# Probabilities turned by VectorE and moved by small transfers, from the thirteenth double on

## What is computed

```python
scores = q @ k.T / 8                  # per batch and head, 576 x 576
# heads 0..3: keys 0..31 back; heads 4..7: every 4th key, 0..124 back
attn = softmax(where(mask, scores, -1e9))
x = attn @ v                          # -> [4, 576, 512]
k = relu(mix(x, mu_k) @ w_k);  v = k * k @ w_v      # mix: with the token before
x = sigmoid(mix(x, mu_r) @ w_r) * v
u = x + (relu(x.T @ w_tok1) @ w_tok2).T             # over the 576 tokens
out = u + relu(u @ w_ch1) @ w_ch2
```

## Time and profile before

| | |
|---|---|
| median of 3 runs | 707.39 us (707.34 to 707.51) |
| profiled execution, its time | 707.65 us |
| profiled execution, its span | 705.9 us |
| TensorE busy | 698.6 us, 99% of the span |
| VectorE busy | 377.5 us, 53% |
| ScalarE busy | 243.2 us, 34% |
| GpSimd busy | 212.8 us, 30% |
| granted TensorE clock | 0.999 of full speed |

### The profile page before, as it was taken

The page is one execution under the profiler, slowest core; times in us unless marked ns, Lnnn a source line. Parts: engine busy times, 40 slices in busy tenths (PEclk is TensorE's granted clock), DMA queues, the critical chain, the costliest instruction groups (busy, mean ns, idle before and its releaser), DMA issues.

```text
span 705.9 us, 13682 instructions
## 1 busy us (share of the span) xinstructions
PE 698.6 (99%) x5469; PEld 624.7 (88%) x5469; DVE 377.5 (53%) x609; ACT 243.2 (34%) x580; POOL 212.8 (30%) x228
## 2 busy tenths in 40 slices
PE   8999999999999999999999999999999999999997
PEld 8878999999999999999988888888788888888886
DVE  6689868687776777776872225321461225411121
ACT  3674563635445463636441122111231122211110
POOL 5584655756464664735045000000000000000000
PEclk9999999999999999999999999999999999999999
DMA  9941333222322220131912221303112121300011
GB/s 176 297 113 35 61 65 73 48 56 48 63 54 48 53 58 24 44 82 23 357 27 41 42 35 59 64 14 66 60 19 48 29 48 59 62 8 0 1 60 30
DMA packets 175695, 45.02 MB, mean 64 GB/s; under 512 B 163848, under 2 KB 168080, under 8 KB 175632
## 3 DMA queue, kind: packets, MB, share of 16 engines
q1 hardware_dynamic: 172192, 43.10, 27.3%
q10 hardware_dynamic: 3440, 1.05, 0.7%
HBM read 29.43 MB, written 4.72 MB: 48 GB/s over the span
## 4 chain that ended last, share of the span: by engine, by line
PE 96%; DVE 2%; issue 0%; ACT 0%; POOL 0%; DVEq 0%; POOLq 0%; ACTq 0%
PE bank L823 12%; PE bank L825 12%; PE bank L824 12%; PE tq L823 8%; PE tq L825 8%; PE tq L824 8%; PE s L1394 4%; PE s L1393 4%; PE s L1392 4%; PE bank L1393 3%; PE bank L1394 3%; PE bank L1392 3%; PE bank L711 3%; PE s L553 3%; PE bank L878 2%; PE bank L659 2%
## 5 line engine op out<-in xcount | busy, mean ns | idle before, releaser
L1384 DVE SCALAR_TENSOR_TENSOR h_lo<-bank,h_hi 128x512 fp32r<-128x512 f32 (+1 forms) x30 | 19.0, 637 | 100.7 <-ACT h_hi L1378 100.6
L1384 DVE SCALAR_TENSOR_TENSOR h_lo<-tq,h_hi 128x512 fp32r<-128x512 f32 (+1 forms) x30 | 18.9, 637 | 98.9 <-ACT h_hi L1378 98.9
L918 POOL TENSOR_TENSOR k_lo<-kr,k_hi 128x288 fp32r<-128x288 f32 x64 | 54.5, 855 | 23.2 <-ACT k_hi L914 22.5
L960 DVE RECIPROCAL rg<-rg 128x288 f32<-128x288 f32 x32 | 61.4, 1920 | 0.0
L1378 ACT ACTIVATE h_hi<-tq 128x512 fp32r<-128x512 f32 (+1 forms) x30 | 16.7, 556 | 118.7 <-PE bank L1394 97.0
L1378 ACT ACTIVATE h_hi<-bank 128x512 fp32r<-128x512 f32 (+1 forms) x30 | 16.7, 556 | 118.0 <-PE bank L1394 93.4
L823 PE MATMUL bank<-k_hi,WV_hi 128*128 128x288 f32 x184 | 56.1, 305 | 0.0
L824 PE MATMUL bank<-k_hi,WV_lo 128*128 128x288 f32 x184 | 54.3, 295 | 0.0
L825 PE MATMUL bank<-k_lo,WV_hi 128*128 128x288 f32 x184 | 54.1, 294 | 0.0
L599 POOL TENSOR_TENSOR sm<-sm,stat 128x640 f32<-128x640 f32 x24 | 30.6, 1277 | 76.8 <-DVE stat L591 76.8
L1394 PE MATMUL s<-C_hi,h_lo 128*128 128x512 f32 x120 | 47.5, 396 | 0.0
(11 more groups left out here) (218 smaller groups left out, 2016.8 us busy)
## 6 DMA issues: line engine op xcount, KB each, us to landing
C_raw<-in_moe_w_ch SPq DMA_DIRECT2D x6, 1024.0 KB, 10.9
urows<-blocks SPq DMA_DIRECT2D x64, 64.0 KB, 2.1
out_x<-urows SPq DMA_DIRECT2D x16, 256.0 KB, 2.1
vt<-in_v SPq DMA_DIRECT2D x40, 80.0 KB, 2.3
qraw<-in_q SPq DMA_DIRECT2D x128, 24.0 KB, 1.8
kraw<-in_k SPq DMA_DIRECT2D x128, 24.0 KB, 1.8
xraw<-blocks SPq DMA_DIRECT2D x48, 64.0 KB, 2.1
vt<-in_v SPq DMA_DIRECT2D x7, 320.0 KB, 3.9
```

The lines of the kernel that those rows point to most:

```text
L918: e.tensor_tensor(lo, t, hi.bitcast(F32), ALU.subtract).then_inc(Z.lo_done, 1)
L960: e.reciprocal(t, t).then_inc(Z.r_done, 1)
L1384: e.scalar_tensor_tensor(lo, ps[:, 0:w], 0.0, hi.bitcast(F32), ALU.max, ALU.subtract).then_inc(Z.h2l_done, 1)
```

## The change

From double 12 on (`NDM`), TensorE's eight transposes of a double's probabilities and ScalarE's four copies are left out. Instead:

- `p_blocks(n)`, in slot start + 7, turns `sm` on VectorE in blocks of 32 by 32, in two instructions (8 x 64 and 8 x 32 columns), to a new buffer `p_turned`. It waits for the normalised probabilities and until all 12 moves of the double before have landed.
- `p_moves` brings the blocks to their rows in `pT`, in 12 transfers from SBUF to SBUF: six from SP (source rows 0 to 31 and 64 to 95), six from ScalarE's queue (rows 32 to 63 and 96 to 127), these in four steps of 2, 1, 2, 1 transfers in the four slots from start(n + 1) + 3 on. Each group waits for `p_blocks(n)` and for the values of double n - 1. In SP's queue the moves of n - 1 stand between `load_v(n)` and `load_blocks(n + 2)`.
- `weighted_values(n)` waits for the landing of the 12 moves and comes 2 slots after the start of double n + 2, one double later than before. 22 and 23 have slots of their own, start + 13.
- `mask(n)` waits, from 14 on, for the block transposes of double n - 2.
- The starts are 5 slots apart up to double 12 (slot 40), 6 up to 17 (slot 70), then 13/2: 23 is at 109.
- The raw q and k blocks and the turned q of double 8 and later get buffers of their own in the space of the old ones; 16 columns behind each turned q are zeroed once, and the block transposes of 8 wait for the scores of 7.

```diff
--- before.py
+++ after.py
@@ -60,6 +60,7 @@
 NU = len(FU)
 TR = 64 + QB
 NPE = 8
+NDM = 12
 
 def ring_user(n, ring, total):
 
@@ -121,9 +122,13 @@
         A0 = o
 
         qraw, kraw = [at(n + "raw", [P, 2 * DM], F32, o + 8 * DM * m) for m, n in enumerate("qk")]
+        W = 2 * SU
+        blocks_in = [[at(f"{n}rows{i}", [P, W], F32, o + 4 * W * (2 * m + i)) for i in range(2)] for m, n in enumerate("qk")]
+        p_turned = at("p_turned", [P, 2 * W], F32, o + 16 * W)
+        qTb = [at(f"qTb{i}", [P, W + 16], F32, o + 24 * W + 4 * (W + 16) * i) for i in range(2)]
         o += 16 * DM
+        qTs = [at(f"qT{i}", [P, 512], F32, o + 2048 * i) for i in range(2)]; o += 4096 + 128
         vts = [at(f"vt{i}", [P, 1024], F32, o + 4096 * i) for i in range(2)]; o += 8192
-        qTs = [at(f"qT{i}", [P, 512], F32, o + 2048 * i) for i in range(2)]; o += 4096
         KTW = [WINDOW + S, DIL * (WINDOW + SUB)]
         kTs = []
         for w in KTW:
@@ -175,7 +180,7 @@
 
         names = """const_done zeroed mu_in mu_turned mu_done
             q_in k_in q_in_a q_in_b q_in_1a q_in_1b k_in_a k_in_b k_in_1a k_in_1b v_in0 v_in1 v_in_2 v_in_3 qk_in0 qk_in1 tq_done tk_done q_done k_done s_done masked max_done sub_done e_done sum_done rc_done nm_done nv_done
-            pa_done pb_done pta_done ptb_done o_done x_done xv_done
+            pa_done pb_done pta_done ptb_done pd_done pt_in o_done x_done xv_done
             difa_done xa_done dif_done xm_done hi_done mix_done
             mm_done relu_done sq_done kh_done lo_done re_done r1_done r_done x2_done
             wk_in0 wk_in1 wk_in2 wk_in3 wr_in wv_in0 wv_in1 wk_hi wk_lo wr_hi wr_lo wv_hi wv_lo_even wv_lo_odd
@@ -405,7 +410,7 @@
 
         def raw_blocks(n):
 
-            return [t[:, DM * (n % 2):DM * (n % 2) + 2 * SU] for t in (qraw, kraw)]
+            return [t[n % 2][:, :] for t in blocks_in]
 
         def load_blocks(n):
 
@@ -429,11 +434,11 @@
         def block_transposes(n):
 
             _, j, dil = where(n)
-            qT, kT = qTs[n % 2], kTs[dil]
+            qT, kT = qTb[n % 2], kTs[dil]
 
             def vector(e):
                 e.wait_ge(qk_in[n % 2], 256 * ((n - NPE) // 2 + 1))
-                wait(e, Z.s_done, n - 1)
+                e.wait_ge(Z.s_done, max(n - 1, NPE))
                 raws = raw_blocks(n)
                 if dil:
                     raws = [r.rearrange("p (s i c) -> p s i c", s=2, c=DIL) for r in raws]
@@ -443,6 +448,8 @@
                     raws = [r.rearrange("p (s t) -> p s t", s=2) for r in raws]
                     dq = qT[:, 0:2 * SU].rearrange("p (s t) -> p s t", s=2)
                     dk = kT[:, :].rearrange("p (s x) -> p s x", s=2)[:, :, WINDOW + SU * j:WINDOW + SU * (j + 1)]
+                if n < NPE + 2:
+                    e.memset(qT[:, W:W + 16], 0.0)
                 e.transpose(dq, raws[0]).then_inc(Z.q_done, 1)
                 e.transpose(dk, raws[1]).then_inc(Z.k_done, 1)
             return dict(vector=vector)
@@ -529,7 +536,7 @@
         def scores(n):
 
             _, j, dil = where(n)
-            qT, kT = qTs[n % 2], kTs[dil]
+            qT, kT = (qTs if n < NPE else qTb)[n % 2], kTs[dil]
 
             def keys(rows, s, c):
                 k0 = (WINDOW + SUB) * (DIL * s + c) + QB * j if dil else (WINDOW + S) * s + QB * (DIL * j + c)
@@ -576,7 +583,9 @@
                 else:
                     m = tiles(masks[:, 0:GC], 4).unsqueeze(1).broadcast_to([P, 2, 4, KB])
                 e.wait_ge(Z.s_done, n + 1)
-                if n >= 4:
+                if n >= NDM + 2:
+                    e.wait_ge(Z.pd_done, 2 * (n - NDM - 1))
+                elif n >= 4:
                     e.wait_ge(Z.pb_done, n - 1 if n >= 6 else n - 3)
                 e.tensor_tensor(sb[:, :].rearrange("p (h g x) -> p h g x", h=2, g=4)[:, :, :, 0:KB],
                                 s2[:, :].rearrange("p (h x) -> p h x", h=2)[:, :, 0:GC].rearrange("p h (g x) -> p h g x", g=4),
@@ -682,6 +691,41 @@
                 e.tensor_copy(dst[:, 1], src[:, :, 64:TR]).then_inc(Z.ptb_done, 1)
             return dict(vector=vector) if h and n in (2, 3) else dict(scalar=scalar)
 
+        P_IN = 16 * 12
+
+        def p_blocks(n):
+
+            sb, _ = soft(n)
+            main_ = p_turned[:, 0:8 * 64].rearrange("p (g x) -> p g x", g=8)
+            rest = p_turned[:, 8 * 64:8 * 96].rearrange("p (g x) -> p g x", g=8)
+            rows = sb[:, :].rearrange("p (g x) -> p g x", g=8)
+
+            def vector(e):
+                e.wait_ge(Z.nm_done, n)
+                wait(e, Z.pt_in, P_IN * (n - NDM))
+                e.transpose(main_, rows[:, :, 0:64]).then_inc(Z.pd_done, 1)
+                e.transpose(rest, rows[:, :, KB - 32:KB]).then_inc(Z.pd_done, 1)
+            return dict(vector=vector)
+
+        def p_move(e, n, r, c):
+
+            i, w = 48 * (r // 2) + 32 * (r % 2), 16 if r % 2 else 32
+            if c < 2:
+                src = p_turned[32 * r:32 * (r + 1), 0:8 * 64].rearrange("p (g x) -> p g x", g=8)[:, :, 32 * c:32 * c + w]
+            else:
+                src = p_turned[32 * r + 16:32 * (r + 1), 8 * 64:8 * 96].rearrange("p (g x) -> p g x", g=8)[:, :, 0:w]
+            dst = pT[32 * c:32 * c + (16 if c == 2 else 32), :].rearrange("p (g x) -> p g x", g=8)[:, :, i:i + w]
+            e.dma_start(dst, src).then_inc(Z.pt_in, 16)
+
+        def p_moves(n, r, cs):
+
+            def queue(e):
+                e.wait_ge(Z.pd_done, 2 * (n - NDM + 1))
+                e.wait_ge(Z.o_done, n)
+                for c in cs:
+                    p_move(e, n, r, c)
+            return dict(sync=queue) if r % 2 == 0 else dict(scalar=queue)
+
         def o_bank(n, s):
 
             if n == 1 or (n, s) == (3, 1):
@@ -693,8 +737,11 @@
         def weighted_values(n):
 
             def tensor(e):
-                e.wait_ge(Z.pta_done, n + 1)
-                e.wait_ge(Z.ptb_done, n + 1)
+                if n < NDM:
+                    e.wait_ge(Z.pta_done, n + 1)
+                    e.wait_ge(Z.ptb_done, n + 1)
+                else:
+                    e.wait_ge(Z.pt_in, P_IN * (n - NDM + 1))
                 e.wait_ge(*v_landed(n))
                 if n in (1, 2, 3):
                     e.wait_ge(Z.k_done, 4)
@@ -988,7 +1035,7 @@
 
 
         UNITS = HP + DT
-        STARTS = [5 * (n - 4) if n <= 9 else 25 + 20 * (n - 9) // 3 for n in range(4, ND)]
+        STARTS = [5 * (n - 4) if n <= NDM else 40 + 6 * (n - 12) if n <= 17 else 70 + 13 * (n - 17) // 2 for n in range(4, ND)]
 
         def flat(units):
             return [s for u_ in units for s in u_]
@@ -1029,8 +1076,11 @@
                      load_weights1(w_v, WV, 4, 4, wv_in[1]), load_weights1(w_r, WR, 0, 4, Z.wr_in)]
             steps += [load_v(5), load_qk(3), load_v(6), load_v(7), load_blocks(8), load_blocks(9)]
             for n in range(8, ND):
-                steps += [load_v(n)] + ([load_blocks(n + 2)] if n + 2 < ND else [])
-            return steps
+                steps += [load_v(n)]
+                if n > NDM:
+                    steps += [p_moves(n - 1, r, range(3)) for r in (0, 2)]
+                steps += [load_blocks(n + 2)] if n + 2 < ND else []
+            return steps + [p_moves(ND - 1, r, range(3)) for r in (0, 2)]
 
         def load_mu():
             def sync(e):
@@ -1077,11 +1127,18 @@
                 early[t + 4].append(exponentials(n))
                 early[t + 5].append(sums(n))
                 late[t + 5].append(normalise(n))
-                late[t + 7].append(p_transpose(n, 0))
-                early[t + 8].append(p_evict(n, 0))
-                late[t + (8 if n < NPE else 7)].append(p_transpose(n, 1))
-                early[t + (9 if n < NPE else 8)].append(p_evict(n, 1))
-                tv = STARTS[n - 3] + 2 if NPE < n < ND - 1 else t + 9
+                if n < NDM:
+                    late[t + 7].append(p_transpose(n, 0))
+                    early[t + 8].append(p_evict(n, 0))
+                    late[t + (8 if n < NPE else 7)].append(p_transpose(n, 1))
+                    early[t + (9 if n < NPE else 8)].append(p_evict(n, 1))
+                    tv = STARTS[n - 3] + 2 if NPE < n else t + 9
+                else:
+                    tv = STARTS[n - 2] + 2 if n < ND - 2 else t + 13
+                    moved = STARTS[n - 3] + 3 if n < ND - 1 else t + 7
+                    late[t + 7].append(p_blocks(n))
+                    for i, (r, cs) in enumerate(((1, (0, 1)), (1, (2,)), (3, (0, 1)), (3, (2,)))):
+                        late[moved + i].append(p_moves(n, r, cs))
                 values[tv].append(weighted_values(n))
                 early[tv + 1].append(x_evict(n))
             for i in range(4):
@@ -1237,7 +1294,7 @@
                         for m_ in range(2):
                             work_free(e, b - 1, "t1", m_)
                     else:
-                        e.wait_ge(Z.ptb_done, ND)
+                        e.wait_ge(Z.ptb_done, NDM)
                         e.wait_ge(Z.x2_done, DT * NU - 1)
```

## The result

The change makes the kernel slower by 3%: 728.88 us as the median of four runs (728.08 to 729.51), against 707.37 us (707.23 to 707.51) for the kernel before in the same job. The ratio is 1.0303, with a 95% interval of 1.0286 to 1.0321. That is outside the predicted range, 15 us beyond its upper end.

What follows compares the result with a forecast made beforehand. TensorE, busy 698.6 of 705.9 us, was taken as the bound. 707.65 - 9.24 (transposes) + 0.4 (blocks standing alone) + 9.9 (waits for SP's queue) = 708.7, as median 708.5 us; range 700.5 to 713.5.

Steps and rivals of the forecast that it cites:

- What TensorE loses and gains: On TensorE: twelve doubles lose 0.77 us of transposes each, 9.24 us; two more blocks standing alone add 0.4 us.
- SP's queue: Moves of 12 to 21: the queue cannot follow, so TensorE waits 9.9 us by the values of 21; chance 0.45.
- 13.6 us a double: SP's issue time per double with six moves of 0.64 us added, against TensorE's 11.54 to 12.3 us.
- the bound: Upper limit of TensorE's waits for SP: 13.3 us, with moves at 0.70 us and 2.3 us to landing.
- What is late next: Section on whether moved probabilities arrive in time; SP's late moves make TensorE wait 9.9 us in sum.
- The earlier starts of 10 to 12: Starts five slots apart leave 10.7 us for SP's 9.8 us a double, so they cost nothing.
- ScalarE, costed at nothing: ScalarE loses four copies, gains six issues: 9.5 of 11.54 us busy a double, with 2.2 us of cover.
- the rival: VectorE sets the pace at its wait for landed moves in start + 7, squares behind it; 714.2 us, chance 0.19.
- The markers: Signs of being right: SP without a wait, TensorE waiting at the values about a microsecond a double, 8 to 12 us.
- my own sign of being wrong: Waits at the values under 3 us, or at products' lines with VectorE as releaser, or moves issued under 0.55 us.
- The rule of the Trainium skill: A DMA's issue time is usually small beside the DMA; by it the sum ends at 698.6 us.

Runs made afterwards that it cites:

- e4: Kernel before with only the new starts, all transposes still on TensorE; 710.84 us, ratio 1.0055 to the kernel before.
- e6: As e5, with the values of doubles 9 to 11 one slot later; 703.94 us, ratio 0.9946 to the kernel before.
- e5: Changed kernel without any of the twelve moves, values waiting for VectorE's block transposes instead; 706.82 us, ratio 0.9984 to the kernel before.
- e1: Changed kernel without the six moves of each double that SP issues; 711.46 us, ratio 1.0059 to the kernel before.
- e2: Changed kernel without the six moves of each double that ScalarE issues; 725.43 us, ratio 1.0251 to the kernel before.
- e3: Changed kernel with the turning of probabilities placed behind the q and k block transposes of its slot; 728.80 us, ratio 1.0304 to the kernel before.
- e9: As e6, with the turning of probabilities placed behind the block transposes of its slot on VectorE; 700.39 us, ratio 0.9904 to the kernel before.
- e7: Changed kernel with two more small transfers in SP's queue for each double from 13 on; 739.72 us, ratio 1.0461 to the kernel before.
- e11: The change for doubles 22 and 23 alone, turning behind the block transposes, starts as in the kernel before; 710.86 us, ratio 1.0053 to the kernel before.

## Why the prediction was wrong

The ladder of ratios, times 707.2 us: 728.6 (the change), 711.4 without SP's moves, 706.1 without any, 703.4 with the values of 9 to 11 a slot later, 700.4 with the turning behind the block transposes. Steps: 17.3, 5.3, 2.7 and 3.0 us. The first two were taken with the stops of the others in place, so they are shares in this order of removal.

The time missed the forecast by 20.4 us (728.9 for 708.5). Three stretches hold it. Ahead of the values of 11, the early starts cost 3.7 us. From the end of the values of 11 (130.6) to the start of the values of 21 (285.5) the kernel took 154.9 us for the predicted 139.3: 15.6 us. Behind them TensorE lost some 3 us more at half clock. That is 22.3 us, 2 us too much; 0.9 of these are a shorter stretch ahead of the scores of 8 in this trace (80.71 for 81.61 before), the rest was not traced.

- **What TensorE loses and gains: right.** 8.8 us; with every wait but one of 0.97 us gone the kernel takes 700.4 us.
- **SP's queue: the right mechanism, priced too low, and the largest miss.** The step that failed is its 13.6 us a double; it takes 14.8 us. The six moves took 3.89 to 4.97 us, 4.2 on average for 3.84; the 16 transfers of blocks 8.85 us for 8.42; v 1.5 for 1.3; the rest is gaps between the groups. From the first move of 12 (141.00) to the last of 21 (279.98) SP needed 139.0 us for the predicted 127.5: 11.5 of the 15.6 us. I had 0.7 us of pauses for the moves of ten doubles. SP also began 0.4 us late. By the start of the values of 21 TensorE was 25.5 us behind (154.9 - 129.4), where I had 9.9 and at most 13.3; the bound let the moves have their highest price but kept the blocks at their old one. Of the 25.5 us, 15.2 stood as waits (11.2 + 4.0) and some 8 as work at half clock.
- **The way from the last move to the values: left out, 3.7 us.** I let the values of 21 begin when their moves landed (281.8). They begin at 285.54, behind VectorE's transposes of 22 and 23 and the scores of 23, these at half clock.
- **The clock: left out, some 5 us.** "What is late next" turned each us of wait into one us of time. The slower clock holds 11 to 13 us of TensorE's busy time, but the 7.4 us inside the stretch that SP sets stand where waits would otherwise stand. On top come 1.7 us behind the early stop (within the 3.7 us of the early starts) and the 3 us or so behind the last one. The windows showed the clock at 1.00 with TensorE never idle, and no row of before had a stop of 4 us within the doubles to show otherwise; the change was going to make some, by my own forecast, and the bound should have held it.
- **The earlier starts of 10 to 12, costed at nothing: wrong**, 3.7 us by e4 (2.7 by e6 against e5). I looked only at whether SP keeps up with five slots, and not at what stands in slot start(n + 1) + 2 when it falls on start(n) + 7.
- **ScalarE, costed at nothing: wrong**, some 5 us with SP's moves gone (e1 against e5), under 4 us with them (e2). Its busy time was right (10.8 us less, 12 x 0.9); its issues come in pairs of 1.25 to 2.4 us in which it does nothing else, and it is late itself, so its moves land late without any queue on SP: in e1 VectorE still waits 8.7 us for them.
- **VectorE: the place of the rival was right, its cause was not.** The wait for landed moves in slot start + 7 does stop TensorE, but what stands behind it is the block transposes of the next double, not a square. And the pace is SP's: e3 moves the waits and leaves the time as it is. I named the square and the mix as what is queued behind, and missed the block transposes, because I followed doubles of six slots and the coincidence needs seven. Without any moves this order still costs 3.0 us (e9 against e6).
- **The markers.** SP without a wait: right, but for 0.4 us. A wait at the values of 8 to 12 us, spread about a microsecond a double: wrong in form. It came in three stops of 4 to 5.6 us, and two of them at the scores with VectorE as the releaser, which is near my own sign of being wrong.
- The rule of the Trainium skill (DMA: Bandwidth & Descriptors, Issuing engines are not separate DMA queues), that time on the issuing sequencer is usually small, fails here further than I had said: e7 shows 0.6 us of time lost per added transfer that moves a kilobyte.

## What to carry to other kernels

Count the instructions of a DMA queue as an engine's work: a step that takes 0.77 us on TensorE and leaves it for twelve transfers buys 7 to 8 us of issue time on two sequencers, and pays only if both have that much free, with some 10% kept for pauses. Where a change can stop TensorE for several microseconds at a time, ask what sets the pace behind the stop: if it is TensorE, add what the slower clock costs (1.7 to 3.7 us a stop here); if it is a queue that is behind anyway, add nothing. When steps are shifted against each other, lay out both cycles and look for slots in which one double's wait stands ahead of another double's first step.

## What was not expected of the hardware

- After a stop of 4.0 to 5.6 us the clock was at 1.2 GHz on return, and for up to 8 us more, with TensorE busy throughout. Of the stops of 1.83 to 1.89 us some were followed by the slower clock and some not. In the profiled runs of seven kernels with the same 1.84 to 1.85 us stop near 117, the window from 116 to 126 shows a clock of 0.83 in four (the changed kernel, e3, e4, e5) and 1.00 in three (e1, e2, e7); in e11 the 1.89 us at 301.39 left it at 1.00. Why one and not the other was not found. Where a median sits a few microseconds high with a wide spread, as in e5 (703.76 to 708.37), this is a likely cause.
- A pair of moves on ScalarE's queue took 1.25 to 2.4 us; a single one took 0.59 to 1.13 us in the changed kernel, and up to 1.87 us in e3. A move on SP's queue took 0.65 us when nothing paused it (six in 3.89), 35% above a transfer of q or k from DRAM (0.48), though both move 32 rows.
- VectorE's second transpose, 256 columns in blocks of 32, took 0.40 us, as estimated.
